# Eight row buffers and earlier gathers for the experts, a dense stage whose first block is turned tile by tile, and constants set in attention's block

## The chip, the cores and the metric

The kernel runs on one core of a Trainium2 chip. The metric is the device time of one execution in microseconds (us), less being better. The core has five engines that run at the same time and meet at semaphores: PE (TensorE, matmuls), DVE (VectorE), ACT (ScalarE), POOL (GpSimd) and SP (SyncE, which here only issues DMAs). DMAs are also issued by ACT and POOL; those with indices (a gather of rows) by POOL alone.

## The reference, cut to what matters

```python
# attention: a recurrence over 768 steps for 4 x 8 heads of 40
y[t]  = r[t] @ state
Sa    = state @ a[t]
state = state * w[t] - outer(Sa, b[t]) + outer(v[t], k[t])
# experts: 3072 tokens of 320 features, each goes to one of 8 experts
logits = x @ w_gate;  e = argmax(logits);  gate = softmax(logits)[e]
x = gate * (relu(x @ w1[e]) @ w2[e])          # w1: 320 x 1024, w2: 1024 x 320
# dense: all tokens
h = x @ w_in;  g = max(h, 0) + alpha * min(h, 0);  out = g @ w_out   # 320 -> 2048 -> 320
```

## The kernel before, in words

There are four blocks one behind another; at the end of each all engines meet, then each engine jumps to its part of the next.

**Constants.** `constants()` is a short block of its own. DVE fills `ones` and `eye`, POOL makes the identity `eye`, the triangles `upper` and `later` out of them, DVE then copies `eye` into `pick`, and SP loads the gate's weights into the rest of `pick` (two DMAs of 5 KB).

**Attention.** SP loads `t_in` (776 KB for each of 48 chunk steps, a ring of `TR` = 3). In the first 24 steps DVE makes running products of `w` (the scans of L406 and L413), then `second` and `alpha`; PE multiplies them, ACT copies the results out, and POOL inverts triangular blocks. The second 24 steps run the recurrence. At its end the router sorts the tokens by expert into 31 tiles of 128 rows (`NET`), `keep.order` holds the rows of each tile, `keep.owner` its expert. POOL gathers the first two tiles before the block ends.

**Experts** (`stage5_experts`). For each of the 31 tiles PE multiplies the tile with `w1` of its expert (24 matmuls, L892), turns the next tile's rows (3 transposes, L880, the helper `transposes`), and multiplies with `w2` (8 matmuls, L905). The rows of a tile come from `gather_x` (L131) into one of `XRING` = 4 buffers `keep.x`; a gather into a buffer in use waits for the transposes of its earlier tile. SP loads `w1` of the tile after next (`load_w1`, in the profile `w<-w_in`, 1024 and 256 KB). POOL's queue holds, in this order: eight loads of `w2` (`load_w2`, 1280 KB each, in the profile `w_all<-w_in`), each behind the landing of the one before, with one gather behind each of the first four (tiles 2 to 5); then tiles 6 to 9; then for each of three pieces `k` of the dense `w_in` a load, a cast and a subtraction on POOL (L863, L864) and four gathers; then the load of `w_out` and the other gathers. PE's loop `Fori` holds `XRING` tiles in a turn; the tiles left over stand behind it.

**Dense** (`stage6_dense`). The tokens go in 6 blocks of 512 (`SUB` = 4 tiles of 128), each against 16 slices of 128 hidden columns. POOL gathers the 24 tiles in the tokens' first order (L993); a gather's rows are 320 wide, so DVE repeats the last 64 columns (`fill`, L1058). PE turns a block in three groups of four transposes (`transposes`, L1007), ACT copies each group as `xt_hi` (L1102), DVE makes the remainder `xt_lo` (L1065), and only then starts `hidden(0)` (8 matmuls of 512 columns, L1020). DVE and ACT work on the hidden part (`neg`, `g`, `g_hi`, `g_lo`), and `outputs(j)` makes 12 matmuls (L1033). Ahead of block 0, ACT and DVE split `w_out` into `w_out_hi` (L1112) and `w_out_lo` (L1074), four pieces each.

Of the kernel before, what the change touches and what calls it, by code (L numbers as in the profile page):

```python
# [15 lines left out]
PARTS = 128  # L16
# [54 lines left out]
def constants(nc, inp, keep):  # L71

    with ExitStack() as ctx:
        m = Memory(nc, ctx)
        s_ones, s_done = m.sem("s_ones"), m.sem("s_const")
        block = ctx.enter_context(nc.Block())

        @block.vector
        def _(dve):
            dve.memset(keep.ones[:, :], 1.0).then_inc(s_ones, 1)  # L80
            dve.memset(keep.eye[:, :], 0.0).then_inc(s_ones, 1)
            dve.wait_ge(s_done, 1)
            for h in HEADS_OF_PAIR:
                dve.tensor_copy(keep.pick[live(h), :, 0:DIM], keep.eye[live(h), HALF * h:HALF * h + DIM].unsqueeze(1).to_broadcast([DIM, QP, DIM]))

        @block.sync
        def _(sp):
            for h in HEADS_OF_PAIR:
                sp.dma_start(keep.pick[live(h), :, DIM:PICK], inp["w_gate"].rearrange("(p h e) n -> h e p n", h=2, e=DIM)[h]).then_inc(keep.s_gw, 16)

        @block.gpsimd
        def _(pool):
            link = chain(pool, s_done)
            pool.wait_ge(s_ones, 2)

            link(pool.affine_select(out=keep.eye[:, :], in_=keep.eye[:, :], compare_op=ALU.not_equal, fill=1.0,
                                    base=0, pattern=[[-1, PARTS]], channel_multiplier=1))

            link(pool.affine_select(out=keep.upper[:, :], in_=keep.ones[:, :], compare_op=ALU.is_gt, fill=0.0,
                                    base=0, pattern=[[1, PARTS]], channel_multiplier=-1))  # L100

            for i in HEADS_OF_PAIR:
                link(pool.affine_select(out=keep.later[rows(i), :], in_=keep.ones[rows(i), 0:C], compare_op=ALU.is_gt,
                                        fill=0.0, base=0, pattern=[[1, C]], channel_multiplier=-1))


AHEAD = 3
XRING = 4
# [62 lines left out]
def attention(nc, inp, dram, keep):  # L171

    with ExitStack() as ctx:
# [47 lines left out]

        s_zero = m_.sem("s_zero_pool")
# [31 lines left out]
        def _(sp):  # L254
# [76 lines left out]
            for j in range(TR):  # L331
                load_t(j)
            for k in range(STEPS):
# [47 lines left out]
        def _(dve):  # L381
            dve.memset(restart[:, :, :], 0.0).then_inc(s_set, 1)
# [3 lines left out]
            dve.memset(yt[:, :, :], 0.0)  # L386
            dve.wait_ge(s_set, 2)
# [163 lines left out]
        def _(pool):  # L551
            for out, pattern, base, step in ((descend, [[-1, EXPERTS]], EXPERTS, 0), (tile_no, [[1, NETS]], 0, 0),
                                             (column, [[1, ET]], 0, 0), (token, [[PARTS, NTT]], 0, 1)):
                pool.iota(out[:, :], pattern=pattern, base=base, channel_multiplier=step,
                          allow_small_or_imprecise_dtypes=True).then_inc(s_iota, 1)
# [93 lines left out]
        def _(pe):  # L649
# [80 lines left out]
            pe.wait_ge(s_bank, 1)  # L730
            for n in ("g1", "bt", "y", "pick"):
                pe.sem_inc(out_of[n], 1)
# [68 lines left out]
def stage5_experts(nc, inp, dram, keep):  # L801
# [3 lines left out]
    with ExitStack() as ctx:  # L805
# [38 lines left out]
        def _(pool):  # L844
            def gather(tile):
                if tile >= XRING:
                    pool.wait_ge(s_t, tile - XRING + 1)
                gather_x(pool, dram, keep, tile)
            for e in range(EXPERTS):
                if e >= 1:  # L850
                    pool.wait_ge(s_w2, 16 * e)
                load_w2(pool, inp, keep, e)
                if e < 4:
                    gather(2 + e)
            pool.wait_ge(s_w2, 16 * EXPERTS)
# [13 lines left out]
            for tile in range(XRING + 6 + 4 * len(KT), NET):  # L869
                gather(tile)  # L870
# [3 lines left out]
        def _(pe):  # L874
# [8 lines left out]
            def body(i, c, tile):  # L883
                s = c % 2
                e = pe.value_load(keep.owner[0:1, ds(tile, 1)], min_val=0, max_val=EXPERTS - 1)
                pe.wait_ge(s_w1[s], 32 * (2 * i + c // 2 + 1))
# [69 lines left out]
def stage6_dense(nc, dram, keep, out):  # L956

    with ExitStack() as ctx:
# [22 lines left out]
        s_gather = [m.sem(f"s_gather6{s}") for s in range(RX)]  # L981
        s_store = [m.sem(f"s_store6{s}") for s in two]
# [5 lines left out]
        def _(pool):  # L988
            for t in range(NTT):
                b = t // SUB  # L990
                if t % SUB == 0 and b >= RX:
                    pool.wait_ge(s_t, NK * (b - RX + 1))
                pool.indirect_dma_start(out=x[b % RX][:, t % SUB, 0:FEAT], out_offset=None, in_=dram["expert_out"],  # L993
                                        in_offset=bass.IndirectOffsetOnAxis(ap=keep.position[:, t:t + 1], axis=0)).then_inc(s_gather[b % RX], 16)
            for s in range(RX):
                pool.wait_ge(s_gather[s], 16 * SUB * NB // RX)

        @block.tensor
        def _(pe):
            def transposes(b, k):  # L1000
                u = NK * b + k
                if k == 0:
                    pe.wait_ge(s_x, b + 1)
                if u >= 2:
                    pe.wait_ge(s_xlo, u - 1)
# [3 lines left out]

            def hidden(j):  # L1010
                b, f = j // NF, j % NF
                if f == 0:
                    pe.wait_ge(s_xlo, NK * (b + 1))
# [25 lines left out]
            for k in range(NK):  # L1039
                transposes(0, k)  # L1040
# [14 lines left out]
        def _(dve):  # L1055
            def fill(b):
                dve.wait_ge(s_gather[b % RX], 16 * SUB * (b // RX + 1))
                dve.tensor_copy(x[b % RX][:, :, FEAT:XW], x[b % RX][:, :, LAST]).then_inc(s_x, 1)  # L1058

            def low_part(b, k):  # L1060
                u = NK * b + k
                part = LOW if KT[k][1] < PARTS else slice(0, PARTS)
                dst = xt_hi if KT[k][1] < PARTS else xt_lo
                dve.wait_ge(s_xt, u + 1)
# [10 lines left out]
            fill(0)  # L1075
            for k in range(NK):
                low_part(0, k)
# [20 lines left out]
        def _(act):  # L1098
            def turned(b, k):
                u = NK * b + k  # L1100
                act.wait_ge(s_t, u + 1)
# [11 lines left out]
            for k in range(NK):  # L1113
                turned(0, k)
# [36 lines left out]
def attention_then_experts(nc, inp, dram, out):  # L1151
    with ExitStack() as ctx:
# [8 lines left out]
        constants(nc, inp, keep)  # L1161
# [7 lines left out]
        keep.x = [m45.sb(f"x5_{s}", [PARTS, FEAT], side="right") for s in range(XRING)]  # L1169
# [4 lines left out]
        keep.w2 = m45.sb("w2_all", [PARTS, EXPERTS * W2], side="right")  # L1174
        keep.w_hi, keep.w_lo = (m.sb(n, [PARTS, len(KT), FF2], F32R) for n in ("w_in_hi", "w_in_lo"))
# [59 lines left out]
```

## Time and profile before

| what | value |
|---|---|
| median of 3 runs | 1150.68 us (1148.93 to 1151.42) |
| the profiled execution, its own time | 1150.59 us |
| its span, first to last instruction | 1148.8 us |
| PE busy | 971.4 us (85%) |
| DVE, ACT, POOL busy | 623.1, 300.8, 328.0 us |
| mean granted clock of PE | 0.981 of full speed |

How to read the rows. A row of the timeline has the start in us, the time from the first start to the last end of what is merged into it, the engine, the line of the kernel, the operation, out<-in, and the count; in brackets how long the engine was idle before it and what ended that. An engine with a small q (SPq, POOLq) is its queue, where DMAs are issued. A row of the chain has the start, the time and the work. A row of windows has the stretch, its length, busy us and count for PE, PE's weight loads, DVE, ACT and POOL, then the granted PE clock (1.00 is 2.4 GHz, 0.50 is 1.2 GHz), the busy share of the 16 DMA engines, and GB/s. A row of the DMA view has the issue, its size and the us to its landing. A matmul in f32 is recorded as two.

### The profile page before, as it was taken

The numbers are of one execution on the slowest core, as the hardware profiler recorded it, in microseconds if no ns is written. First come the engines' busy times: TensorE is split into PE (matmuls) and PEld (weight loads), VectorE is DVE, ScalarE is ACT, GpSimd is POOL, SyncE is SP. The second block draws the span as 40 slices with busy tenths as digits, with TensorE's granted clock in tenths as the row PEclk, the third lists the DMA queues.
The fourth block names the chain that finished last, engine by engine and source line by source line (L and its number), as shares of the span: only waits on it lengthen the run. The fifth ranks groups of instructions, "written<-read, shape, count | busy, mean of one in ns | idle before, by whom it ended". The sixth has DMA issues, their size and how long they took to land. (4 is left out here: it accounts for less than half of the span.)

```text
span 1148.8 us, 44183 instructions
## 1 busy us (share of the span) xinstructions
PE 971.4 (85%) x19549; PEld 869.4 (76%) x19550; DVE 623.1 (54%) x991; ACT 300.8 (26%) x697; POOL 328.0 (29%) x411
## 2 busy tenths in 40 slices
PE   2412339999999988959999999977999999999997
PEld 2402339888988966848888888866999989999996
DVE  7999976888887762101111111115666656666654
ACT  4412433555555510000000000011222222221211
POOL 1682998898920002123332100004101000000000
PEclk9999999999999998979999999997999999999999
DMA  6733774788887636974666745413000100000000
GB/s 213 224 85 103 205 232 146 235 242 248 247 249 238 187 110 224 298 236 145 208 202 178 254 159 151 145 67 86 24 23 18 29 1 24 1 24 1 20 5 23
DMA packets 114614, 158.26 MB, mean 138 GB/s; under 512 B 59092, under 2 KB 87652, under 8 KB 114180
## 3 DMA queue, kind: packets, MB, share of 16 engines
q1 hardware_dynamic: 104276, 127.28, 36.5%
q0 software_dynamic: 5824, 25.28, 7.6%
q10 hardware_dynamic: 4464, 5.08, 1.3%
q8 instruction: 26, 0.43, 0.2%
q14 instruction: 24, 0.20, 0.1%
HBM read 131.98 MB, written 19.23 MB: 132 GB/s over the span
## 5 line engine op out<-in xcount | busy, mean ns | idle before, releaser
L927 DVE TENSOR_SCALAR ht<-h_bank 128x512 f32<-128x512 f32 x62 | 42.9, 691 | 282.8 <-PE h_bank L892 282.8
L892 PEld LDWEIGHTS h_bank<-xt,w 128*128 128x128 f32 x1488 | 172.9, 194 | 8.2 <-issue 3.4
L892 PE MATMUL h_bank<-xt,w 128*128 128x128 f32 x1488 | 173.2, 277 | 3.2 <-issue 3.2
L661 PE MATMUL bank<-alpha,second 40*64 40x64 f32 x1568 | 45.0, 270 | 114.3 <-DVE alpha L420 114.3
L905 PE MATMUL y_bank<-w_all,ht 128*128 x496 | 140.6, 437 | 0.0
L1124 ACT CAST g_hi<-g 128x512 fp32r<-128x512 f32 x96 | 59.5, 620 | 279.8 <-DVE g L1085 279.8
L661 PEld LDWEIGHTS bank<-alpha,second 40*64 40x64 f32 x1568 | 39.1, 179 | 116.8 <-issue 116.8
L163 POOL TENSOR_TENSOR solved<-solved,share 128x31 f32<-128x31 f32 (+15 forms) x155 | 118.6, 765 | 12.2
L1033 PE MATMUL y_bank<-w_out_hi,g_hi 128*128 128x320 f32 x384 | 119.3, 311 | 1.9 <-DVE g_lo L1070 1.9
L905 PEld LDWEIGHTS y_bank<-w_all,ht 128*128 128x128 f32 x496 | 93.1, 193 | 35.2 <-issue 1.4
L160 POOL TENSOR_TENSOR share<-solved,blk 128x31 f32<-128x31 f32 (+15 forms) x155 | 115.9, 748 | 12.2
L1033 PE MATMUL y_bank<-w_out_hi,g_lo 128*128 128x320 f32 x384 | 118.7, 309 | 0.0
L1033 PE MATMUL y_bank<-w_out_lo,g_hi 128*128 128x320 f32 x384 | 118.5, 309 | 0.0
L1020 PE MATMUL h_bank<-xt_hi,w_in_hi 128*128 128x512 f32 x288 | 114.9, 399 | 1.4 <-DVE xt_hi L1065 1.4
L1020 PE MATMUL h_bank<-xt_hi,w_in_lo 128*128 128x512 f32 x288 | 113.5, 394 | 0.0
L1081 DVE TENSOR_SCALAR neg<-h_bank,slope 128x512 f32<-128x512 f32 x96 | 72.0, 750 | 70.9 <-PE h_bank L1020 70.7
L131 POOL DMA_INDIRECT x<-x_rows_mid,order x31 | 30.1, 971 | 256.9 <-PE t_bank L880 136.0
L1070 DVE TENSOR_TENSOR g_lo<-g,g_hi 128x512 fp32r<-128x512 f32 x96 | 66.5, 692 | 65.8 <-ACT g_hi L1124 65.8
L1033 PEld LDWEIGHTS y_bank<-w_out_hi,g_hi 128*128 128x128 f32 x384 | 72.1, 188 | 6.7 <-DVE g_lo L1070 2.6
L1020 PE MATMUL h_bank<-xt_lo,w_in_hi 128*128 128x512 f32 x192 | 76.1, 396 | 0.0
L1033 PEld LDWEIGHTS y_bank<-w_out_lo,g_hi 128*128 128x128 f32 x384 | 72.1, 188 | 3.1
L1033 PEld LDWEIGHTS y_bank<-w_out_hi,g_lo 128*128 128x128 f32 x384 | 72.1, 188 | 0.0
(161 smaller groups left out, 1591.5 us busy)
## 6 DMA issues: line engine op xcount, KB each, us to landing
w<-w_in SPq DMA_DIRECT2D x31, 1024.0 KB, 5.3
t_in<-wab_in SPq DMA_DIRECT2D x24, 776.0 KB, 7.1
t_in<-wak_in SPq DMA_DIRECT2D x24, 776.0 KB, 5.5
w_all<-w_in POOLq DMA_DIRECT2D x8, 1280.0 KB, 8.7
rr<-rr_in SPq DMA_DIRECT2D x24, 384.0 KB, 3.3
w<-w_in SPq DMA_DIRECT2D x31, 256.0 KB, 6.4
vt<-vt_in SPq DMA_DIRECT2D x24, 256.0 KB, 3.2
vtm<-vtm_in SPq DMA_DIRECT2D x24, 240.0 KB
```

What stands on the lines that cost most here:

```text
L131: pool.indirect_dma_start(out=keep.x[tile % XRING][:, :], out_offset=None, in_=dram["x_rows"], in_offset=bass.IndirectOffsetOnAxis(ap=keep ...
L160: link(eng.tensor_tensor(part, q[:, 0:j + 1, j:j + 1].to_broadcast(shape), h[:, j:j + 1, j + 1:B].to_broadcast(shape), ALU.mult))
L163: link(eng.tensor_tensor(rest, rest, part, ALU.subtract))
L661: last = pe.matmul(out[HALF * to:HALF * to + rows_out, row, n * i:n * i + n], lhs, rhs, start=opens and i == 0, stop=closes and i == HP - 1)
L892: last = pe.matmul(h_bank[s][f // FH][:, f % FH * ET:(f % FH + 1) * ET], w1[s][:, k, f * PARTS:(f + 1) * PARTS], xt[s][:, k, :], start=k = ...
L905: last = pe.matmul(y_bank[s][:, 0:FEAT], ht[s][:, f, :], w2[:, ds(e * W2 + f * FEAT, FEAT)], start=f == 0, stop=f == NF - 1)
L927: dve.tensor_scalar(ht[s][:, FH * n:FH * n + FH, :].rearrange("q f t -> q (f t)"), h_bank[s][n][:, :], 0.0, None, ALU.max).then_inc(s_relu, 1)
L1020: last = pe.matmul(h_bank[j % 2][:, :], w[:, k, f * PARTS:(f + 1) * PARTS], x_part[b % 2][:, k, :], start=n == 0, stop=n == len(passes) - 1)
L1033: last = pe.matmul(y_bank[n][:, 0:FEAT], g_part[j % RING][:, n * PARTS:(n + 1) * PARTS], v[:, f, :], start=f == 0 and p == 0, stop=f == NF ...
L1070: dve.tensor_tensor(g_lo[j % RING][:, :], g[j % 2][:, :], g_hi[j % RING][:, :].bitcast(F32), ALU.subtract).then_inc(s_glo, 1)
L1081: dve.tensor_scalar(neg[j % 2][:, :], h_bank[j % 2][:, :], 0.0, keep.slope[:, f:f + 1], ALU.min, ALU.mult).then_inc(s_neg, 1)
L1124: act.copy(g_hi[j % RING][:, :], g[j % 2][:, :]).then_inc(s_ghi, 1)
```

## The change

The constants' block is gone; its work stands at the head of attention's block, and SP loads the gate's weights behind its first three loads of `t_in`. `XRING` is 8. POOL's gathers of tiles 2 to 9 stand between the loads of `w2`: two behind each of the first three, one behind the fifth and one behind the seventh; the gathers behind them follow as before with other numbers. In the dense stage the first block is turned by tiles: each of its four gathers has a semaphore of its own, PE turns the three pieces of one tile into a bank of `y_bank`, ACT copies them with one instruction, DVE makes the remainder with two. PE begins the dense stage with eight matmuls whose results are not used (`idle(8)`).

```diff
-def constants(nc, inp, keep):
...
-XRING = 4
+XRING = 8
...
             for j in range(TR):
                 load_t(j)
+            for h in HEADS_OF_PAIR:
+                sp.dma_start(keep.pick[live(h), :, DIM:PICK], ...).then_inc(keep.s_gw, 16)
...
+            dve.memset(keep.ones[:, :], 1.0).then_inc(s_ones, 1)
+            dve.memset(keep.eye[:, :], 0.0).then_inc(s_ones, 1)
             dve.memset(restart[:, :, :], 0.0).then_inc(s_set, 1)
...
+            dve.wait_ge(s_const, 4)
+            for h in HEADS_OF_PAIR:
+                dve.tensor_copy(keep.pick[live(h), :, 0:DIM], ...)
...
+            EARLY = ((2, 3), (4, 5), (6, 7), (), (8,), (), (9,), ())
...
-                if e < 4:
-                    gather(2 + e)
+                for tile in EARLY[e]:
+                    gather(tile)
             pool.wait_ge(s_w2, 16 * EXPERTS)
-            for tile in range(XRING + 2, XRING + 6):
-                gather(tile)
...
-                for tile in range(XRING + 6 + 4 * k, XRING + 10 + 4 * k):
+                for tile in range(XRING + 2 + 4 * k, XRING + 6 + 4 * k):
                     gather(tile)
...
+            def first_transposes(n):
+                pe.wait_ge(s_x, n + 1)
+                for k in range(NK):
+                    last = pe.transpose(y_bank[n][:, k * PARTS:(k + 1) * PARTS], x[0][:, n, KT[k][0]:KT[k][0] + PARTS], keep.eye[:, :])
+                last.then_inc(s_t, 1)
+
+            def idle(count):
+                for _ in range(count):
+                    pe.matmul(h_bank[0][:, :], keep.ones[:, :], keep.w_out[:, 0:2, 0:256], start=True, stop=True)
...
-            for k in range(NK):
-                transposes(0, k)
+            idle(8)
+            for n in range(SUB):
+                first_transposes(n)
             hidden(0)
             hidden(1)
...
-            fill(0)
-            for k in range(NK):
-                low_part(0, k)
+            first_fill(0)
+            for n in range(SUB):
+                if n + 1 < SUB:
+                    first_fill(n + 1)
+                first_low(n)
```

On POOL, at the head of the experts' block, this is the order before (`w_all` is `w2`, `x_3` is buffer 3 of `keep.x`, `s_t5` counts the tiles that PE has turned, `s_w2` the landings of `w2`):

```order
L125 DMA w_all<-w_in 128x8x320
L131 DMA x_2<-x_rows_mid,order 128x320
L125 DMA w_all<-w_in 128x8x320 [waits s_w2]
L131 DMA x_3<-x_rows_mid,order 128x320
L125 DMA w_all<-w_in 128x8x320 [waits s_w2]
L131 DMA x_0<-x_rows_mid,order 128x320 [waits s_t5]
L125 DMA w_all<-w_in 128x8x320 [waits s_w2]
L131 DMA x_1<-x_rows_mid,order 128x320 [waits s_t5]
L125 DMA w_all<-w_in 128x8x320 [waits s_w2] x4
L131 DMA x_2<-x_rows_mid,order 128x320 [waits s_t5,s_w2]
```

and the same place on POOL after:

```order
L89 DMA w_all<-w_in 128x8x320
L95 DMA x_2<-x_rows_mid,order 128x320
L95 DMA x_3<-x_rows_mid,order 128x320
L89 DMA w_all<-w_in 128x8x320 [waits s_w2]
L95 DMA x_4<-x_rows_mid,order 128x320
L95 DMA x_5<-x_rows_mid,order 128x320
L89 DMA w_all<-w_in 128x8x320 [waits s_w2]
L95 DMA x_6<-x_rows_mid,order 128x320
L95 DMA x_7<-x_rows_mid,order 128x320
L89 DMA w_all<-w_in 128x8x320 [waits s_w2] x2
L95 DMA x_0<-x_rows_mid,order 128x320 [waits s_t5]
L89 DMA w_all<-w_in 128x8x320 [waits s_w2] x2
```

The last row before is tile 6, behind all eight loads; after, tile 6 is `x_6`, behind three, and `x_0` is tile 8.

On DVE, at the head of the dense block, before (`s_gather60` is the landing of all four tiles of block 0):

```order
L1074 TENSOR_TENSOR w_out_lo<-w_out_sb,w_out_hi 128x1280 [waits s_vhi6] x4
L1058 COPY x_0<-x_0 128x4x64 [waits s_gather60]
L1065 TENSOR_TENSOR xt_lo<-t_bank,xt_hi 128x512 [waits s_xt6] x2
L1065 TENSOR_TENSOR xt_hi<-t_bank,xt_hi 64x512 [waits s_xt6]
L1081 TENSOR_SCALAR neg_0<-h_bank,slope 128x512 [waits s_h6]
```

and after (`s_first60` to `s_first63` are the landings of the single tiles):

```order
L1081 TENSOR_TENSOR w_out_lo<-w_out_sb,w_out_hi 128x1280 [waits s_vhi6] x4
L1053 COPY x_0<-x_0 128x64 [waits s_first60]
L1053 COPY x_0<-x_0 128x64 [waits s_first61]
L1058 TENSOR_TENSOR xt_lo<-y_bank,xt_hi 128x2x128 [waits s_xt6]
L1060 TENSOR_TENSOR xt_hi<-y_bank,xt_hi 64x128
L1053 COPY x_0<-x_0 128x64 [waits s_first62]
L1058 TENSOR_TENSOR xt_lo<-y_bank,xt_hi 128x2x128 [waits s_xt6]
L1060 TENSOR_TENSOR xt_hi<-y_bank,xt_hi 64x128
L1053 COPY x_0<-x_0 128x64 [waits s_first63]
```

Four instructions have become twelve smaller ones, and they still stand behind the four pieces of `w_out_lo`; PE has its eight extra matmuls at this place.

## Rows read from the trace of the kernel before

**Rows 1.** The page: the span.

```profile
span 1148.8 us, 44183 instructions
```

**Rows 2.** The page's summary of the chain that ended last, then pieces of the chain.

```profile
PE h_bank L1020 15%; PE y_bank L1033 14%; PE t_bank L1007 1%; POOL x L993 0%; DMA x<-expert_out_mid,position 0%; ACT y L1109 0%; DVE neg L1081 0%; DVE g_lo L1070 0%; DVE g L1085 0%; ACT g_hi L1124 0%; ACT xt_hi L1102 0%; DVE xt_hi L1065 0%; DVE xt_lo L1065 0%; DVE x L1058 0%; POOLq L805 0%
...
777.13 3.08 DMA x<-expert_out_mid,position
...
785.61 3.79 PE h_bank L1020 x8
792.34 2.03 PE y_bank L1033 x12
794.37 1.84 PE h_bank L1020 x8
```

**Rows 3.** Timeline of PE in the experts' block: the first tile, and tiles 5 to 7.

```profile
441.23 7.61 PE L892 MATMUL h_bank<-xt,w 128*128 128x128 f32 x48 [3.17 <-issue]
...
493.29 5.52 PE L892 MATMUL h_bank<-xt,w 128*128 128x128 f32 x48
...
512.40 0.90 PE L880 MATMUL t_bank<-eye,x 128*128 128x128 f32 x3 [13.59 <-DMA x<-x_rows_mid,order]
...
519.40 5.52 PE L892 MATMUL h_bank<-xt,w 128*128 128x128 f32 x48
...
529.39 5.52 PE L892 MATMUL h_bank<-xt,w 128*128 128x128 f32 x48
```

**Rows 4.** Timeline of POOL in the experts' block.

```profile
498.99 0.88 POOL L125 DMA_DIRECT2D w_all<-w_in  x1 [8.39 <-DMA w_all<-w_in]
509.14 1.00 POOL L131 DMA_INDIRECT x<-x_rows_mid,order  x1 [9.26 <-DMA w_all<-w_in]
...
521.09 4.62 POOL L864 TENSOR_TENSOR w_in_lo<-w_raw,w_in_hi 128x2048 fp32r<-128x2048 f32 x1
```

**Rows 5.** Timeline at the program's start.

```profile
0.80 0.78 SPq L89 DMA_DIRECT2D pick<-w_gate_in  x2
...
3.23 9.11 SPq L264 DMA_DIRECT2D t_in<-wab_in  x4
...
7.79 1.26 DVE L406 TENSOR_TENSOR_SCAN suf<-t_in,restart 128x528 f32<-128x528 f32 x1 [2.87 <-DMA t_in<-wab_in]
...
11.90 1.25 DVE L406 TENSOR_TENSOR_SCAN suf<-t_in,restart 128x528 f32<-128x528 f32 x1
```

**Rows 6.** Timeline at the head of the dense block.

```profile
771.82 4.74 ACT L1112 CAST w_out_hi<-w_out_sb 128x1280 fp32r<-128x1280 f32 x4 [2.27 <-PEq L805]
...
773.11 5.70 DVE L1074 TENSOR_TENSOR w_out_lo<-w_out_sb,w_out_hi 128x1280 fp32r<-128x1280 f32 x4 [7.60 <-ACT w_out_hi L1112]
...
780.23 0.29 DVE L1058 COPY x<-x 128x256 f32<-128x256 f32 x1 [1.43 <-DMA x<-expert_out_mid,position]
780.58 1.97 PE L1007 MATMUL t_bank<-eye,x 128*128 128x128 f32 x8 [11.49 <-DVE x L1058]
...
784.25 0.58 ACT L1102 CAST xt_hi<-t_bank 128x512 fp32r<-128x512 f32 x1 [1.08 <-PE t_bank L1007]
784.86 0.69 DVE L1065 TENSOR_TENSOR xt_hi<-t_bank,xt_hi 64x512 fp32r<-64x512 f32 x1 [0.97 <-ACT xt_hi L1102]
```

**Rows 7.** Windows of half a microsecond around the clock's fall and rise.

```profile
773.00:773.50 0.50, 0.00 (x0) 0.00 (x0) 0.39 (x1) 0.50 (x2) 0.43 (x1) 0.61 0.00 0
...
790.00:790.50 0.50, 0.50 (x3) 0.41 (x2) 0.47 (x2) 0.00 (x0) 0.50 (x1) 0.82 0.35 72
```

**Rows 8.** Timeline: the nine extra matmuls of attention's end.

```profile
419.27 7.89 PE L728 MATMUL bank<-t_in,ones 128*128 128x512 f32 x18
```

**Rows 9.** Windows of tiles 2 to 5, then the DMA view of 457 to 467 us.

```profile
457.00:497.00 40.00, 40.00 (x271) 34.94 (x270) 5.53 (x8) 3.80 (x12) 4.62 (x5) 1.00 0.95 299
...
w<-w_in SPq DMA_DIRECT2D x1, 256.0 KB, 9.8
```

**Rows 10.** Timeline of PE where attention's second loop begins a turn.

```profile
258.64 0.22 PE L661 MATMUL bank<-swt,alpha 40*64 40x40 f32 x1 [0.84 <-DMA ax<-alpha]
```

More of the change, by code:

```diff
@@ L68, in chain @@
     return link
-def constants(nc, inp, keep):
[L73 to L104, printed above, removed]
 AHEAD = 3
-XRING = 4
+XRING = 8
 W2 = FF1 // PARTS * FEAT
@@ L551, in _ @@
         def _(pool):
+            pool.wait_ge(s_ones, 2)
+            link = chain(pool, s_const)
+            link(pool.affine_select(out=keep.eye[:, :], in_=keep.eye[:, :], compare_op=ALU.not_equal, fill=1.0,
+                                    base=0, pattern=[[-1, PARTS]], channel_multiplier=1))
+            link(pool.affine_select(out=keep.upper[:, :], in_=keep.ones[:, :], compare_op=ALU.is_gt, fill=0.0,
+                                    base=0, pattern=[[1, PARTS]], channel_multiplier=-1))
+            for i in HEADS_OF_PAIR:
+                link(pool.affine_select(out=keep.later[rows(i), :], in_=keep.ones[rows(i), 0:C], compare_op=ALU.is_gt,
+                                        fill=0.0, base=0, pattern=[[1, C]], channel_multiplier=-1))
             for out, pattern, base, step in ((descend, [[-1, EXPERTS]], EXPERTS, 0), (tile_no, [[1, NETS]], 0, 0),
@@ L868, in _ @@
             pool.dma_start(keep.slope[:, :], inp["slope"]).then_inc(s_dense, 16)
-            for tile in range(XRING + 6 + 4 * len(KT), NET):
+            for tile in range(XRING + 2 + 4 * len(KT), NET):
                 gather(tile)
@@ L981, in stage6_dense @@
         s_gather = [m.sem(f"s_gather6{s}") for s in range(RX)]
+        s_first = [m.sem(f"s_first6{n}") for n in range(SUB)]
         s_store = [m.sem(f"s_store6{s}") for s in two]
@@ L1055, in _, with first_fill, first_low @@
         def _(dve):
+            def first_fill(n):
+                dve.wait_ge(s_first[n], 16)
+                dve.tensor_copy(x[0][:, n, FEAT:XW], x[0][:, n, LAST]).then_inc(s_x, 1)
+            def first_low(n):
+                part = slice(n * PARTS, n * PARTS + PARTS)
+                dve.wait_ge(s_xt, n + 1)
+                dve.tensor_tensor(xt_lo[0][:, 0:NK - 1, part], y_bank[n][:, 0:(NK - 1) * PARTS].rearrange("q (k c) -> q k c", c=PARTS),
+                                  xt_hi[0][:, 0:NK - 1, part].bitcast(F32), ALU.subtract)
+                dve.tensor_tensor(xt_hi[0][LOW, NK - 1, part], y_bank[n][LOW, (NK - 1) * PARTS:NK * PARTS],
+                                  xt_hi[0][LOW, NK - 1, part].bitcast(F32), ALU.subtract).then_inc(s_xlo, 1)
             def fill(b):
-                dve.wait_ge(s_gather[b % RX], 16 * SUB * (b // RX + 1))
+                dve.wait_ge(s_gather[b % RX], 16 * SUB * (b // RX + (b % RX > 0)))
                 dve.tensor_copy(x[b % RX][:, :, FEAT:XW], x[b % RX][:, :, LAST]).then_inc(s_x, 1)
             def low_part(b, k):
-                u = NK * b + k
+                u = NK * (b - 1) + k
                 part = LOW if KT[k][1] < PARTS else slice(0, PARTS)
                 dst = xt_hi if KT[k][1] < PARTS else xt_lo
-                dve.wait_ge(s_xt, u + 1)
+                dve.wait_ge(s_xt, SUB + u + 1)
                 dve.tensor_tensor(dst[b % 2][part, k, :], t_bank[u % 2][part, :], xt_hi[b % 2][part, k, :].bitcast(F32),
@@ L1112, in _ @@
                 act.copy(v_hi[:, part, :], keep.w_out[:, part, :]).then_inc(s_vhi, 1)
-            for k in range(NK):
-                turned(0, k)
+            for n in range(SUB):
+                act.wait_ge(s_t, n + 1)
+                act.copy(xt_hi[0][:, :, n * PARTS:(n + 1) * PARTS], y_bank[n][:, 0:NK * PARTS].rearrange("q (k c) -> q k c", c=PARTS)).then_inc(s_xt, 1)
             for j in range(NB * NF):
@@ L1168, in attention_then_experts @@
         keep.w1 = [m45.sb(f"w1_{s}", [PARTS, len(KT), FF1], side="right") for s in (0, 1)]
-        keep.x = [m45.sb(f"x5_{s}", [PARTS, FEAT], side="right") for s in range(XRING)]
+        keep.x = [m45.sb(f"x5_{s}", [PARTS, FEAT], side="right") for s in (0, 1)]
         keep.s_w1 = [m45.sem(f"s_w1{s}") for s in (0, 1)]
@@ L1174, in attention_then_experts @@
         keep.w2 = m45.sb("w2_all", [PARTS, EXPERTS * W2], side="right")
+        keep.x += [m45.sb(f"x5_{s}", [PARTS, FEAT], side="right") for s in range(2, XRING)]
         keep.w_hi, keep.w_lo = (m.sb(n, [PARTS, len(KT), FF2], F32R) for n in ("w_in_hi", "w_in_lo"))
```

26 lines of the change are left out of this document (15 added, 11 removed).

## The prediction

> **What bounds the kernel now.** I read the page first: the span is 1148.8 us [rows 1] and the execution's own time 1150.59, so 1.8 us lie around the span. The median of the runs is 1150.68, 0.1 us from the profiled one, so the sum can be made on the profile and read as a median. Then the chain that ended last: it is PE almost alone, the two matmul lines of the dense stage [rows 2]. It goes back no further than the gathers at that stage's head, so it says what an idle piece there is worth (all of it) and nothing about what came before. The blocks follow one another, and PE's timeline takes over: in the experts' block a tile takes 529.39 - 519.40 = 9.99 us, and PE is never idle in that time; but tile 5 starts at 493.29 and tile 6 at 519.40 [rows 3]. In between PE was idle for 13.59 us, until the rows of tile 6 had landed. POOL's timeline says why they were late: the eighth load of `w2` is issued at 498.99, POOL waits for its landing, and the gather of tile 6 goes out at 509.14 [rows 4]. In the dense stage's head I read who waits for whom: the gathered rows land at 780.2 (777.13 + 3.08 [rows 2]), DVE fills, PE turns, ACT and DVE copy, and the first product starts at 785.61 [rows 2, 6]. The windows tell the granted clock there: it drops at about 773.1, four us after PE's last matmul (780.58 - 11.49 = 769.09 [rows 6]), and comes back at about 790.2 [rows 7].
>
> **Part 1, gathers and eight buffers: -16.1 us.** What is removed is not only the 13.59 us. From the start of tile 5 to that of tile 6 are 26.11 us where 9.99 are normal [rows 3]: 16.1 us are lost, the 2.5 us above the wait being the matmuls behind it at half clock. After the change tile 6 is gathered behind the third load of `w2`, that is (five loads of about 9.3 us before 498.99 [rows 4]) at about 453, and is needed at about 499. Tiles 8 and 9 wait for the transposes of tiles 0 and 1, long done, and stand behind the fifth and the seventh load; they are needed at 519 and 529 in the time of before, so also not late. Where the stall could go is next: tile 10 stands behind the eighth landing (509.1) and the first piece of `w_in`, whose work on POOL ended at 521.09 + 4.62 = 525.7 before, with four gathers ahead of it (1.00 and some 0.3 to the next, 5 us in all) that are gone now [rows 4]: 521 to 522. It is needed when tile 9 is multiplied, about 493.3 + 4 x 10 + 5.4 = 539. That is 17 us of slack, against 3 to 10 us that a gather takes to land. The following groups of four come as early or earlier. The eight buffers themselves cost no time; the gathers are the same in number.
>
> **Part 2, constants: -2.4 us.** The first `t_in` load is issued at 3.23, and DVE starts on it at 7.79 [rows 5]. Now that load is SP's first work, where the small loads stood at 0.80: 2.43 us earlier. DVE had been idle for 2.87 us when the load came, so its own memsets ended at 4.92, 1.7 us after SP's issue at 3.23; with the small block's work, which fitted with its waits between 0.8 and 3.2, in front of them, it is ready by 4.9, before 5.4, when the data is there. The two small loads go behind the three large ones, and SP then waits for DVE anyway. DVE sets the pace of the first 24 steps (4.1 us each, back to back [rows 5]), and the recurrence follows it, so I carry all of it to the end. Bounds: nothing, if something else starts attention; 2.43 at most.
>
> **Part 3, the dense stage's head: -3.0 us.** (a) The extra matmuls. Nine such took 7.89 us at full clock [rows 8], eight take 7.0; no row shows when PE enters this block, ACT enters at 771.82 [rows 6], so they end at about 778.8. At half clock all the way they would take 14, until 785.8, and PE would be late: that is the upper bound. (b) The tiles. DVE is busy with `w_out_lo` until 773.11 + 5.70 = 778.81 [rows 6], so the first fill can't come before; the early landing of tile 0 is worth little. From there: fill 0.2, three transposes 0.4 to 0.7 (eight took 1.97 at half clock), the copy 0.58 x 3/4 = 0.4, the remainder 0.69 x 3/4 and a second instruction, 0.65 [rows 6]. DVE's order is fill 0, fill 1, low 0, fill 2, low 1, fill 3, low 2, low 3. Low 0 ends at 780.7, fill 2 at 780.9, low 1 at 781.5, fill 3 at 781.7 (its rows landed at 780.2), then transposes to 782.1, copy to 782.6, low 3 to 783.3. The first product starts at about 783.5 instead of 785.61: 2.1 us. (c) The clock. Eight matmuls took 3.79 us there and 1.84 two pieces later [rows 2]. From the first product's start to the first of `outputs` were 792.34 - 785.61 = 6.7 us; at full clock the first eight end 1.9 us sooner, and the rest of that stretch is DVE and ACT, so up to 1.9 more. If the clock is down, nothing of it. I take half, 0.9, because no row shows whether the clock stays up over sparse transposes; it fell after four idle us [rows 6, 7], and the transposes leave PE idle for more than half of the 4.7 us before the first product. Together 3.0, between 3.9 and, with the extra matmuls at half clock to the end, a loss: tiles turned from 785.8, first product at about 790, 4.4 us late, 1.9 of them given back by the clock, +2.5.
>
> **The sum.** 1148.8 - 16.1 - 2.4 - 3.0 = 1127.3, and 1.8 around it: 1129.1 us.
>
> **The rivals.** *The head of the dense stage gives nothing.* The extra matmuls run partly at half clock and the tiles are no faster, since DVE has twelve instructions where it had four. For it: the 2.7 us without PE work before them, and DVE's place behind `w_out_lo`. Then 1150.6 - 18.5 = 1132.1. Against it: the clock was still at full at 773, later than they begin [rows 7].
>
> *The longer loop stalls.* PE's loop turn goes from four tiles to eight, with three jumps back. In the rows the four-tile loop shows none (9.99 us a tile across jumps), and attention's second loop, whose turn has about as many matmuls as eight tiles, shows 0.84 us at the start of a turn, which the profile puts down to a DMA [rows 10]. At 0.84 a jump: 2.5 us, 1131.6. The Trainium skill, Runtime: NRT & Kernel Launch, section Instruction fetch mechanics, speaks for it: a taken branch to code no longer held must wait for a fetch; no row here shows such a stall by itself, and by the rows' price the time would be that 1131.6, by none 1129.1.
>
> *The blocks' merger gives nothing:* what stood in the small block holds the start up, or the first load of the program is slow whatever it carries. 1131.5.
>
> *The stall stays, at a later tile.* A group behind a piece of `w_in` comes late and costs the same 16.1: 1145.2. The 17 us of slack speak against.
>
> *Slower: the loads of `w1` come late.* The four gathers moved ahead are 4 x 160 KB, about 2.2 us of the DMA engines at the 299 GB/s of tiles 2 to 5, when these are 95% busy; the small part of `w1` took 9.8 us to land there [rows 9]; it is issued some 6 us after a tile's start and needed at the start of the tile after next, 20 us after it, so it has about 4 us left. Every tile under the loads of `w2`, seven of them, would have to lose on; to end above 1153 it must eat 24 us, 3.4 a tile, which takes landings of about 17 us. The Trainium skill, Trainium Kernel Development and Optimization, section Key Constraints, has all queues interleave on the same 16 engines, and the long landings at 95% agree; but 2.2 us in all is not 24.
>
> **How the numbers follow.** Chances: the forecast with its own range 1126 to 1131.4, 0.80; the dense head gives nothing 0.08; the loop 0.04; the merger 0.03; the stall stays 0.03; slower 0.01; and 0.01 that it cancels to no change. Downward, 0.9 more from the clock in part 3, and the 2.1 us that the first tile now loses at half clock (7.61 against 5.52 [rows 3]), which an earlier or later rise can give back: 1126.1. Upward, the two middle rivals, 1132.1, and a bit of two together: 1133. Within 0.2% (about 2.3 us, what a measurement of this kernel can tell from no change) I give 0.01, slower 0.01, faster 0.98.
>
> **What would show it.** Right: PE idle nowhere in the experts' block, tile starts 9.99 us apart from tile 1 to 30; the first scan at about 5.4; the first product of the dense stage 14.3 to 14.5 us behind the experts' last matmul (16.5 before), at granted clock 1.00. Wrong: a gap at tiles 8, 16, 24 (the loop) or at 10, 14 or 18 (a gather behind POOL's work); clock 0.50 under the extra matmuls, or PE still in them when the first fill is done; `w1` landing more than 13 us after issue.

## The result and the profile after

The changed kernel takes 1133.62 us (median of 4, 1132.11 to 1135.17) against 1151.05 us beside it; the ratio is 0.9847, 95% interval 0.982 to 0.9873. That is faster by 1.5%, as forecast, but 4.5 us above the forecast of 1129.1 and 0.6 us above the end of the range. The profiled execution has a span of 1131.5 us and a time of 1133.65, so 2.2 us lie around the span, where 1.8 lay before.

One profile against the other, by the blocks' landmarks (first scan; first product of tile 0; last matmul of the experts; first product of the dense stage; first matmul of `outputs`; end):

| stretch, us | before | after | difference |
|---|---|---|---|
| start to first scan | 7.79 | 5.49 | -2.30 |
| first scan to tile 0's product | 433.44 | 434.93 | +1.49 |
| experts' block from there | 327.86 | 311.68 | -16.18 |
| its end to the dense stage's first product | 16.52 | 16.31 | -0.21 |
| first product to first of outputs | 6.73 | 6.57 | -0.16 |
| from there to the end | 356.5 | 356.5 | 0.0 |

The start, where [rows 5] stood before: SP's first work is now the load of `t_in`, and DVE begins 2.30 us sooner.

```profile
0.80 1.35 SPq L229 DMA_DIRECT2D t_in<-wab_in  x3
...
5.49 1.26 DVE L378 TENSOR_TENSOR_SCAN suf<-t_in,restart 128x528 f32<-128x528 f32 x1 [2.19 <-DMA t_in<-wab_in]
```

PE's timeline at tiles 5, 6 and 8 and POOL's at the gathers of tiles 6 and 10 answer to [rows 3, 4]. Tile 6 is turned at once behind tile 5's product, at full clock (0.49 us, before 0.90), and there is no gap. Tile 8 starts at 522.36. From tile 1 to tile 30 all starts are 9.99 to 10.03 us apart, across the jumps of the loop and under all loads.

```profile
492.38 5.52 PE L874 MATMUL h_bank<-xt,w 128*128 128x128 f32 x48
497.74 0.49 PE L862 MATMUL t_bank<-eye,x 128*128 128x128 f32 x3
...
522.36 5.52 PE L874 MATMUL h_bank<-xt,w 128*128 128x128 f32 x48
```

```profile
452.58 0.98 POOL L95 DMA_INDIRECT x<-x_rows_mid,order  x1 [0.30 <-issue]
...
509.81 0.56 POOL L843 DMA_DIRECT2D w_raw<-w_in_in  x1 [10.36 <-DMA w_all<-w_in]
...
523.48 1.04 POOL L95 DMA_INDIRECT x<-x_rows_mid,order  x1 [0.28 <-POOL w_in_lo L846]
```

The dense stage's head, where [rows 6] stood:

```profile
754.82 4.74 ACT L1121 CAST w_out_hi<-w_out_sb 128x1280 fp32r<-128x1280 f32 x4 [2.26 <-PEq L787]
754.85 8.80 PE L1002 MATMUL h_bank<-w_out_sb,ones 128*128 128x512 f32 x16 [2.75 <-PEq L787]
...
756.11 5.70 DVE L1081 TENSOR_TENSOR w_out_lo<-w_out_sb,w_out_hi 128x1280 fp32r<-128x1280 f32 x4 [7.59 <-ACT w_out_hi L1121]
...
761.73 0.29 DVE L1053 COPY x<-x 128x64 f32<-128x64 f32 x2
...
763.49 0.82 PE L997 MATMUL y_bank<-eye,x 128*128 128x128 f32 x6
...
765.54 0.55 PE L997 MATMUL y_bank<-eye,x 128*128 128x128 f32 x3 [1.23 <-DVE x L1053]
...
766.53 0.55 PE L997 MATMUL y_bank<-eye,x 128*128 128x128 f32 x3 [0.44 <-DVE x L1053]
...
768.41 0.60 PE L1014 MATMUL h_bank<-xt_hi,w_in_hi 128*128 128x512 f32 x1 [1.34 <-issue]
...
774.98 0.41 PE L1027 MATMUL y_bank<-w_out_hi,g_hi 128*128 128x320 f32 x1 [1.04 <-issue]
```

The fills are ready at 762.0, but PE is in the extra matmuls until 763.5. Half-microsecond windows (columns as in [rows 7]) say why these took 8.80 us and not 7.0, and why the first products are hardly faster than before:

```profile
755.00:755.50 0.50, 0.50 (x1) 0.17 (x2) 0.00 (x0) 0.50 (x1) 0.00 (x0) 0.52 0.00 0
...
758.00:758.50 0.50, 0.50 (x2) 0.26 (x1) 0.50 (x1) 0.50 (x2) 0.42 (x1) 0.57 0.00 0
...
768.50:769.00 0.50, 0.50 (x2) 0.40 (x3) 0.00 (x0) 0.00 (x0) 0.40 (x1) 0.67 0.64 195
...
772.00:772.50 0.50, 0.50 (x4) 0.42 (x3) 0.46 (x1) 0.00 (x0) 0.50 (x1) 0.92 0.81 174
```

The granted clock falls to 0.50 when the extra matmuls have just begun, after PE's idle time from the experts' end, and is there until 758.4. It falls again at 768.7, just as the first product starts, after five microseconds in which PE had only the transposes.

### The profile page after: what moved, and what is told of

The parts are those of the page before. It is cut to its first block and busy times, and to the rows that moved or that the text cites. A ratio compares the mean times of both kernels' runs of the same rounds, so it can differ in the third digit from the quotient of the medians.

```text
span 1131.5 us, 44178 instructions
## 1 busy us (share of the span) xinstructions
PE 976.8 (86%) x19565; PEld 870.8 (77%) x19566; DVE 625.4 (55%) x999; ACT 301.0 (27%) x698; POOL 326.5 (29%) x411
## 5 line engine op out<-in xcount | busy, mean ns | idle before, releaser
L976 POOL DMA_INDIRECT x<-expert_out_mid,position x24 | 23.9, 995 | 189.6 <-POOLq L787 96.1
```

## The experiments

Sixteen runs were made: ten variants, two of them repeated, and the changed kernel twice more. Where an interval stands, each was timed in five rounds beside the kernel before on the same chip. The times of this kernel scatter widely: 49 executions of the kernel before, run from 1143.58 to 1158.55 us with a mean of 1150.1 and a standard deviation of 3.4 (eleven more, beside `e_keep_b` and `e_best2_b` in the last set of runs, have a mean of 1153.7), and 16 of the changed kernel from 1127.96 to 1140.74 with a mean of 1133.0. So sizes under 3 us are read from the landmarks in the profiles, and times only confirm sums.

### Each part alone

`e_gathers` is the kernel before with the eight buffers and the new order of gathers:

```diff
-XRING = 4
+XRING = 8
...
-                if e < 4:
-                    gather(2 + e)
+                for tile in EARLY[e]:
+                    gather(tile)
```

> Only the experts' block is changed (eight buffers, gathers between the loads of w2). Both theories: tile 6 no longer waits, the block is 16 us shorter, nothing else moves: 1151 - 16 = 1135 us, tiles 9.99 us apart also at 8, 16 and 24. If a jump of the longer loop cost anything, tiles 8, 16, 24 would start late.

Measured: ratio 0.9859 (0.9824 to 0.9894), 1135.03 us; the experts' block 312.2 us from tile 0's product (before 327.9). PE's timeline at tiles 7 and 8, across the first jump back of the loop:

```profile
515.58 5.52 PE L892 MATMUL h_bank<-xt,w 128*128 128x128 f32 x48
...
525.57 5.52 PE L892 MATMUL h_bank<-xt,w 128*128 128x128 f32 x48
```

Tile 8 starts 9.99 us after tile 7. The part is worth its 16 us, and the jump costs nothing. Buffers and order were changed together, so it is not shown that the eight buffers are needed: before, PE turned tile 2, which frees the buffer of tile 6, at 458.67, so that a gather of tile 6 behind the fifth load (473.21) might have been in time with four buffers too. No run tests that.

`e_const` is the kernel before with the constants in attention's block:

```diff
-        constants(nc, inp, keep)
...
             for j in range(TR):
                 load_t(j)
+            for h in HEADS_OF_PAIR:
+                sp.dma_start(keep.pick[live(h), :, DIM:PICK], ...).then_inc(keep.s_gw, 16)
```

> Only the constants are moved into attention's block. Theory 1 (the start's lead of 2.3 us is kept, and the changed kernel's profile lost it in one recurrence step of 14.8 us at half clock, by chance): first scan at 5.49, median 2 us below before, about 1149. Theory 2 (the recurrence catches up whatever the start gains): first scan at 5.49 all the same, but attention's end within 0.8 us of before, median 1151.

Measured: ratio 0.9982 (0.9955 to 1.0009), mean of 12 1147.7 us against 1150.0 of 23. First scan at 5.41, tile 0's product at 440.68, 0.55 us ahead of the kernel before. The mean is what theory 1 has, the one profile is what theory 2 has; the landmarks of all profiles tell a little more (below).

`e_dense` is the kernel before with the new head of the dense stage, its extra matmuls with it:

```diff
-            for k in range(NK):
-                transposes(0, k)
+            idle(8)
+            for n in range(SUB):
+                first_transposes(n)
```

> Only the dense head is changed, with its eight extra matmuls. Theory 1 (the head's gain is eaten by the extra matmuls running partly at half clock and by the clock's fall before the first product): from the experts' last matmul to the first of outputs 22.9 us where before has 23.2, so about 0.4 us gained: 1150.6. Theory 2 (my sum: 3.0 us, and the profile of the changed kernel met an unlucky moment of the clock): 1148, with the clock at full from the first product on.

Measured: ratio 0.9969 (0.9945 to 0.9993). Experts' end to first product 16.33 us, from there to outputs 5.76: 22.1 against 23.2 before. The clock again fell under the extra matmuls, and once more 1.2 us after the first product started, so the 3.0 of my sum was not there in this profile either: 1.2. Two windows around that second fall:

```profile
784.00:785.00 1.00, 1.00 (x5) 0.81 (x5) 0.00 (x0) 0.00 (x0) 0.70 (x2) 0.99 0.34 113
785.00:786.00 1.00, 1.00 (x5) 0.71 (x4) 0.00 (x0) 0.00 (x0) 0.70 (x2) 0.50 0.44 143
```

Theory 1 has the mechanism; how much of the first products is at full clock differs from profile to profile (5.76, 6.57, 6.46, 6.21 us in four profiles at this head). The times alone lean to theory 2: the mean of 12 is 1146.8 us, 3.1 below the kernel before, and the interval is 0.8 to 6.3 us. `e_olddense` is the second test.

`e_olddense` is the changed kernel with the dense stage of before (`transposes(0, k)`, no extra matmuls).

> The changed kernel with the dense stage of before: the gathers and the constants alone. Theory 1 (the new dense head gives 0.4 us): 1133, the same as the changed kernel within a us. Theory 2 (the three parts disturb each other, as the single runs' sum of some 21 us against 17 could mean): this one is as fast as or faster than the changed kernel, 1130.

Measured: 1133.33 us, ratio 0.9839 (0.9808 to 0.9871), beside the changed kernel's 0.9844 (0.9802 to 0.9886) in the same set of runs. Head 16.44 and 6.72. Beside the changed kernel the new head gives nothing that these times can tell (means 1132.6 and 1132.5), as theory 1 has it.

### The changed kernel again

`e_again` and `e_again2` are the changed kernel without an edit.

> The changed kernel once more. Theory 1: the long recurrence step is chance, so this profile has it elsewhere or not at all; without it the span is some 1126. Theory 2: it is part of this kernel, at the same step, about 282 us, and costs 5 us again; 1133.6.

> The changed kernel a third time, beside the others of this call. Both theories: head 16.3 us and 5.8 to 6.7 to outputs, experts' block 311.7, attention anywhere between 425 and 433 us; median 1131 to 1134.

Measured: 1132.1 us, ratio 0.9858 (0.9822 to 0.9893), and 1130.62 us. The long recurrence step was in neither profile; the spans are 1128.8 and 1127.5. Theory 1 said some 1126 without it: right in kind, 1.5 to 3 us too low.

### The head of the dense stage

`e_noidle` is the changed kernel without the line `idle(8)`.

> The changed kernel without the eight extra matmuls. Theory 1 (they end 1.5 us after DVE's first fill and the clock is down at the first product all the same, so they cost): from the experts' last matmul to the first product 15.3 us instead of 16.3, then 6.7 to outputs as before; some 0.8 us faster than with them. Theory 2 (they are what keeps the head from being slower): head of 17 us or more.

Measured (one profile): first product 15.60 us behind the experts' end, 6.73 to outputs: 22.3, where the changed kernel has 22.9. Its timeline:

```profile
760.01 0.29 DVE L1052 COPY x<-x 128x64 f32<-128x64 f32 x2
...
760.25 1.54 PE L997 MATMUL y_bank<-eye,x 128*128 128x128 f32 x6 [9.88 <-DVE x L1052]
...
765.97 0.80 PE L1014 MATMUL h_bank<-xt_hi,w_in_hi 128*128 128x512 f32 x1 [1.33 <-DVE xt_hi L1059]
```

PE follows the fill at once, but at half clock (1.54 us for six transposes, with the extra matmuls 0.82). The four profiles with the eight matmuls in this place have 22.9, 22.8, 22.5 and 22.1 us in all, so the matmuls give nothing that shows, and cost at most 0.6: theory 1, and less than its 0.8.

`e_early` moves DVE's work and has no extra matmuls:

```diff
-            for n in range(4):
...
-            first_fill(0)
+            low_v(0)
+            first_fill(0)
+            low_v(1)
             for n in range(SUB):
...
+            low_v(2)
+            low_v(3)
```

(`low_v(n)` makes piece n of `w_out_lo`.)

> The changed kernel without the extra matmuls, and with DVE's order in the dense head changed: fill 0 behind the first piece of w_out_lo, the other fills and remainders behind the second, the last two pieces at the end. Theory 1 (DVE's place behind w_out_lo is what holds the tile-by-tile turning back): first product 13.3 us behind the experts' last matmul where the changed kernel has 16.3; clock still at half in it, 6.7 to outputs. Theory 2 (the landing of the gathers bounds the head): 15 us or more.

Measured (one profile): 14.49 us to the first product, 6.74 to outputs, 21.2. 1.1 us better than `e_noidle` and 1.2 short of the expectation: DVE now waits for the rows.

```profile
765.01 0.20 DVE L1052 COPY x<-x 128x64 f32<-128x64 f32 x1 [1.56 <-DMA x<-expert_out_mid,position]
...
766.34 0.20 DVE L1052 COPY x<-x 128x64 f32<-128x64 f32 x1 [0.38 <-DMA x<-expert_out_mid,position]
```

So each theory has a part: `w_out_lo` held the head, and with it out of the way the landing of tiles 2 and 3 does.

`e_spread` leaves DVE as in the change and spreads the extra matmuls:

```diff
-            idle(8)
+            idle(5)
             for n in range(SUB):
                 first_transposes(n)
+                idle(1)
```

> The changed kernel with five extra matmuls ahead of the first tile and one behind each tile's transposes, DVE's order as in the change. Theory 1 (the clock falls because PE is mostly idle between the transposes): the clock stays at full, first product at 16.0 us or less and 4.8 to outputs instead of 6.6, 2 us gained. Theory 2 (the clock falls whatever stands there): 6.6 again.

Measured (one profile): 15.33 and 5.06, 20.4 in all, 2.5 us less than in the changed kernel's profile, with nine extra matmuls for its eight. PE's timeline, and a window that has the clock:

```profile
756.16 6.23 PE L1002 MATMUL h_bank<-w_out_sb,ones 128*128 128x512 f32 x10 [2.76 <-PEq L787]
763.29 0.55 PE L997 MATMUL y_bank<-eye,x 128*128 128x128 f32 x3 [0.90 <-DVE x L1054]
763.67 1.02 PE L1002 MATMUL h_bank<-w_out_sb,ones 128*128 128x512 f32 x2
...
768.73 0.50 PE L1014 MATMUL h_bank<-xt_hi,w_in_hi 128*128 128x512 f32 x1 [0.47 <-DVE xt_hi L1061]
```

```profile
764.00:765.00 1.00, 1.00 (x6) 0.61 (x5) 0.60 (x2) 0.35 (x1) 0.76 (x1) 1.00 0.34 77
```

The clock is back at 1.00 at 760.4, under the first five, and stays there. What made it fall a second time in the changed kernel was PE's sparse work between the transposes: theory 1. All four profiles with the extra matmuls in one piece have that second fall, 0.3 to 1.2 us behind the start of the first product; none of the eight profiles with them spread has it there.

`e_best` has DVE's order of `e_early`, `idle(3)` ahead and `idle(1)` behind each tile.

> The changed kernel with DVE's new order, three extra matmuls ahead and one behind each tile. Theory 1: both gains add: first product at 13.5 us, 4.8 to 6.7 to outputs, so 18.3 to 20.2 from the experts' last matmul to outputs where the changed kernel has 22.9 and before 23.2; time 3 to 4.5 us below the changed kernel, about 1129. Theory 2: the gathers or the clock bound it, no more than 1 us.

Measured: 1127.81 us, ratio 0.9817 (0.9779 to 0.9856). Head 14.09 and 5.82, but 358.0 us from there to the end instead of 356.5. DVE's two late pieces hold the first `neg` back to 763.52, though the product's eight matmuls were through at 762.6; PE waits, and the clock falls behind that wait:

```profile
760.57 2.91 DVE L1082 TENSOR_TENSOR w_out_lo<-w_out_sb,w_out_hi 128x1280 fp32r<-128x1280 f32 x2
...
763.52 0.75 DVE L1095 TENSOR_SCALAR neg<-h_bank,slope 128x512 f32<-128x512 f32 x1
...
766.42 0.42 PE L1027 MATMUL y_bank<-w_out_hi,g_hi 128*128 128x320 f32 x1 [1.88 <-DVE g_lo L1078]
```

```profile
765.00:766.00 1.00, 0.00 (x0) 0.00 (x0) 0.32 (x1) 0.62 (x1) 0.70 (x2) 1.00 0.57 164
...
767.00:768.00 1.00, 1.00 (x5) 1.00 (x5) 0.72 (x2) 0.21 (x1) 0.69 (x2) 0.50 0.14 26
```

`e_best2` is made to mend both (the extra matmuls write `t_bank`, which nobody uses yet), and `e_best2_b` is the same kernel once more:

```diff
                 first_low(n)
+                if n == 0:
+                    low_v(2)
-            low_v(2)
             low_v(3)
...
             hidden(0)
             hidden(1)
+            idle(1)
```

> As the one with both gains, but DVE makes the third piece of w_out_lo while it waits for tile 2, only the fourth at the end, and one extra matmul stands ahead of the first outputs. Theory 1 (DVE's two late pieces held the first neg up by 0.9 us, and PE's wait there let the clock fall again, 1.6 us): first product to outputs 4.9 to 5.1 us, from there to the end 356.5; 19.1 from the experts' last matmul to outputs. Theory 2: the piece moved ahead delays the gathers of tiles 2 and 3 and the head gets a us longer: no gain over the run before.

Measured: 1128.89 us, ratio 0.9802 (0.9772 to 0.9833); in the second set of runs 0.98 (0.9754 to 0.9846). Head 14.01 and 5.07, 19.08 in all: what was expected, and 3.8 us less than in the changed kernel's profile. PE's timeline and a window:

```profile
760.51 4.36 PE L1002 MATMUL t_bank<-w_out_sb,ones 128*128 128x512 f32 x6 [2.76 <-PEq L787]
...
771.76 0.50 PE L1014 MATMUL h_bank<-xt_hi,w_in_hi 128*128 128x512 f32 x1 [0.47 <-DVE xt_hi L1062]
...
776.83 0.41 PE L1027 MATMUL y_bank<-w_out_hi,g_hi 128*128 128x320 f32 x1 [0.26 <-DVE g_lo L1079]
```

```profile
775.00:776.00 1.00, 1.00 (x6) 0.61 (x4) 0.39 (x1) 0.57 (x1) 0.69 (x2) 1.00 0.24 92
```

From there to the end it is 356.5 us in one profile and 357.4 in the other. Of the six profiles with this head (the four of `e_keep` below among them) four have the longer value; in `e_best2_b` PE is idle in it for 0.67 us, 11.7 us behind the first of outputs, and why is open:

```profile
782.22 0.41 PE L1027 MATMUL y_bank<-w_out_hi,g_hi 128*128 128x320 f32 x1 [0.67 <-DVE g_lo L1079]
```

This is the shortest head; what the moved piece and the added matmul each give is not separated. The intervals of its time and the changed kernel's still overlap, because attention's scatter is larger than the gain.

### Attention's scatter

The changed kernel's profile shows a recurrence step of 14.8 us. The clock fell in it at 284.0, behind a window in which PE was busy for 0.77 of 2.00 us, and then stood at half while PE was busy all the time. The same group of matmuls takes 1.08 us in it and 0.66 later:

```profile
282.00:284.00 2.00, 0.77 (x47) 0.80 (x49) 1.37 (x3) 0.00 (x0) 1.84 (x3) 0.99 0.96 366
288.00:290.00 2.00, 2.00 (x75) 1.92 (x72) 0.49 (x1) 0.41 (x1) 1.76 (x4) 0.50 0.00 0
```

```profile
291.57 1.08 PE L642 MATMUL bank<-rr,st 40*40 40x64 f32 x32
...
399.64 0.66 PE L642 MATMUL bank<-rr,st 40*40 40x64 f32 x32
```

`e_keep` is `e_best2` with one small matmul at the start of each turn; `e_keep_b`, `e_keep_c` and `e_keep_d` repeat it, beside `e_best2_b`:

```diff
             with pe.Fori(1, STEPS + 1) as i:
+                pe.matmul(BA[:, 0, 0:PARTS], keep.ones[:, :], keep.ones[:, :], start=True, stop=True)
                 arrive(s_ax, 32 * i)
```

> As the run before, with one extra matmul of 128 columns at the start of each turn of the recurrence, ahead of the wait for ax. Theory 1 (the scatter of attention comes from half-clock stretches that begin at such a wait): no half-clock stretch in the recurrence, attention at 428 us or less, spread of the times under 4 us. Theory 2 (the matmul costs more than it holds, or the stretches begin elsewhere): attention 430 us or more, stretches as before.

> The kernel with one extra matmul a turn of the recurrence, again. Theory 1 (half-clock stretches of the recurrence make attention's scatter, and the extra matmul holds them off): no stretch again, from the first scan to the experts' first product 427 to 431 us. Theory 2 (the look without a stretch was luck, as 7 of 13 looks without the matmul had none): a stretch in this look or the next two.

> The same once more, one look. Theory 1: no stretch. Theory 2: as likely as not one.

> The same once more, one look. Theory 1: no stretch. Theory 2: as likely as not one.

> The kernel without that matmul beside them, again. Theory 1: times scatter wider than with it and their mean is 1 us above. Theory 2: no difference.

Measured: `e_keep` 1128.38 us, no stretch at half clock, spread 5.5 us; `e_keep_b` 1134.56 us, with 10 us at half clock in the recurrence; the two further profiles had none. Beside them `e_best2_b` took 1130.01 us with 7 us at half clock. So the matmul doesn't hold the stretches off; theory 1 of these runs falls.

What the 14 profiles without that matmul show (first scan to the experts' first transpose, in us): seven in which the clock column has no half-clock stretch 429.8, 431.5, 428.0, 428.6, 430.0, 425.3, 427.4, mean 428.7; seven with one 431.2, 431.6, 433.5, 431.9, 430.3, 436.1, 431.0, mean 432.2. The longest stretch, in `e_spread`, lasted from 180 to 207 us:

```profile
190.00:192.00 2.00, 2.00 (x96) 2.00 (x92) 1.54 (x3) 1.55 (x5) 1.92 (x2) 0.50 0.62 187
```

A stretch goes with 3.5 us more, but within each group about 6 us of scatter remain. That is because the larger part of the half clock is not in the clock column, which prints 1.00 from the program's start on. The same groups of matmuls tell otherwise: the matmuls of 40 x 64 take 311 ns in every profile up to a moment between 177 and 209 us, and 218 ns behind it, as in and behind the later stretches. The profile's clock entries begin at that moment, and the time ahead of them is counted as full, in the mean granted clocks too (0.981 before). In `e_best2`, the longest attention of the 14, the timeline and a window:

```profile
191.73 1.08 PE L642 MATMUL bank<-rr,st 40*40 40x64 f32 x32
...
206.31 1.08 PE L642 MATMUL bank<-rr,st 40*40 40x64 f32 x32
...
226.25 0.66 PE L642 MATMUL bank<-rr,st 40*40 40x64 f32 x32
```

```profile
206.00:208.00 2.00, 2.00 (x96) 2.00 (x92) 1.70 (x3) 1.55 (x5) 1.84 (x3) 1.00 0.80 197
```

In `e_best`, the shortest, the clock is up before 188:

```profile
188.25 0.66 PE L642 MATMUL bank<-rr,st 40*40 40x64 f32 x32
...
197.78 0.66 PE L642 MATMUL bank<-rr,st 40*40 40x64 f32 x32
```

A step of the recurrence takes 14.58 us at half clock (191.73 to 206.31) and 9.53 at full (188.25 to 197.78), so each us at half clock costs 0.35 us. From the first scan to that first rise, and in the stretches behind it, the clock is at half for 177.6 us in all in `e_best` and for 210.0 in `e_best2`. Over the 14 profiles the length of attention follows this sum with a correlation of 0.93 and a slope of 0.34, and of its scatter (standard deviation 2.7 us) 1.0 is left. So attention's scatter is in the main the clock: first when it rises, then whether it falls again. The four profiles with the extra matmul lie 2.3 to 3.4 us above that line, which is an estimate of what the matmul costs; `e_keep` was short because its clock rose at 177. Why the rise comes early or late no run shows.

## Why the prediction was right and where it was wrong

**Part 1, the gathers: right, 16.1 forecast, 16.2 measured** (15.6 alone). Tile 10, named as next in danger, had its gather issued at 523.48 and was turned by PE at about 537.7, behind the product of tile 9: 14 us, where I had counted 17. With starts 9.99 to 10.03 us apart from tile 1 on, no tile waited for rows or for `w1`, which answers the rivals of the later stall and of the late loads; the landings of `w1` the profile doesn't tell. The rival of the longer loop is out: in the part's profile tile 8 starts 9.99 us behind tile 7, across a jump of the eight-tile loop. The rule of the Trainium skill (Runtime: NRT & Kernel Launch, Instruction fetch mechanics) that spoke for that rival showed no effect in this row; whether the jump left the code that was held, no row here shows.

**Part 2, the constants: the start right, 2.30 of 2.4 us; the step that failed is "I carry all of it to the end".** Through the first 24 steps it is carried: before, the 24th scan starts at 147.85 us, after at 145.96, in the fourteen other profiles with the new start at 144.5 to 145.8, in the two others with the old one at 147.2 and 147.6. (The reason that I gave holds only in part: 4.1 us is the distance of the first eight scans; over the 24 steps the mean is 6.1, so DVE isn't back to back all through.) Behind that the recurrence scatters by more than the lead. In the profile after, 1.5 us of it are gone at the experts' start; in `e_again` the lead there is 3.4. In the mean of eleven profiles with the new start and without `e_keep`'s matmul, tile 0 is turned at 436.1 us, in the three with the old one at 437.6, so 1.5 us are left, with a standard deviation of 3 us from profile to profile. `e_const` is 2.2 us below before in the mean of 12 and 23 runs, but its interval holds zero. That the lead reaches the end is likely and not shown.

**Part 3, the dense head, is most of the miss (2.6 of the 4.5 us): wrong, 3.0 forecast, 0.4 measured (1.2 in the part alone, by the landmarks).** Three steps failed, the second mostly through the first. (a) "Eight take 7.0 at full clock" took 8.80: I had read the clock as full when they begin, which it was, and not asked whether it would fall under them because of the idle time just before. The granted clock was 0.50 from 755.0 to 758.4, and PE was 1.5 us late for DVE's fills. (b) "The first product starts at about 783.5", 2.1 us sooner, became 0.2: besides those 1.5 us, the 4.5 us that I had from the fills to the first product were 4.9. (c) "I take half, 0.9" of the clock became 0.16: the clock fell again behind the sparse transposes. The rival that the head gives nothing, by the clock under the extra matmuls and by DVE's place, was nearly the case; I gave it 0.08, and its 1132.1 is 1.5 us below the measured median. `e_spread` shows that 1.7 of the 1.9 us of the clock are to be had (5.06 for 6.73), and `e_early`, `e_best` and `e_best2` that DVE's order holds 1.1 to 1.3 more, which I had noted ("DVE's place behind `w_out_lo`") without making it the price.

**The range** left out the scatter between executions. The 4.5 us between forecast and time are 2.6 of part 3, 1.5 that attention took longer from its first scan on, 0.1 at the start, and 0.4 around the span: I had carried over the 1.8 us of before as fixed, and they are 2.2. That is so in every run of the changed kernel and of its variants, `e_olddense` too, while the kernel before and each part alone have 1.7 to 1.9; so it comes with the gathers and the constants together, and why is open. With part 3 at its measured 0.4 my sum would have been 1131.7. Over all 16 runs of the changed kernel the mean is 1133.0, and the difference of means to before is 17.1 us where the measured parts add to 18.9 (16.2, 2.3, 0.4), less the 0.4 around the span 18.5. The 1.4 us between these are within what the scatter (3.4 us in one execution, on either side) leaves open. Whether the change lets the half-clock stretches behind the first rise come more often (none in three profiles with the old start, seven in eleven with the new one) is open too; three profiles are too few.

## What to carry to other kernels

A stall behind a queue is priced by the distance of two starts around it, not by the wait: 26.1 - 10.0 us held the wait and the half-clock work behind it, and came back whole. Matmuls that are to hold the clock belong between the sparse pieces of work, where PE would idle, not in one lump ahead of them, where they can only be late; five ahead and one behind each of four tiles did what eight in one lump did not. Where a kernel's time scatters, compare the length of one and the same group of matmuls over time before trusting the clock column: here it showed half clock up to 177 to 209 us where the column has 1.00. Before tiles are handed over one by one, look at what stands ahead of the first of them on the engine that takes them: here four pieces of other work did, and two of them could wait.

## What the runs showed of the hardware

PE can be at half clock for 27 us in one piece while its records fill every microsecond: in the recurrence of `e_spread` the clock that had fallen to its lower level (1.2 of 2.4 GHz) stood there from 180 to 207 us. From the program's start PE was at the lower level until 177 to 209 us, in all 18 profiles, by the same matmuls of 40 x 64, which take 311 ns before and 218 behind; the profile's clock column doesn't show this stretch. Under the extra matmuls of the changed kernel's head the lower level lasted from 755.0 to 758.4. So a full PE row does not say that the clock is full: the same group of the recurrence takes 1.08 us at the one level and 0.66 at the other, and where a stretch is longer than its work explains, the granted clock of that stretch and the length of a known group in it are to be read together.
